# Tail scores moved next to the next pair's first scores, with a new order in the early pairs

## The chip, the cores and the metric

The kernel runs on one core of a Trainium2 chip. The metric is the device time of one execution in microseconds. TensorE (PE), VectorE (DVE), ScalarE (ACT) and GpSimd (POOL) each run their own instruction stream in order; SyncE (SP) issues the DMAs. Streams wait for each other by semaphores alone.

## What is computed

Attention with a memory over 4 x 8 heads of 576 rows and 64 columns, then two expert layers on the 2304 rows of 512, all in float32:

```python
scores = scale * q @ k.T, causal;  a = softmax(scores)
local = a @ v
mem_out = (phi(q) @ M_prev) / (phi(q) @ z_prev + 1e-6)
x = g * mem_out + (1 - g) * local          # rows x 512 over the heads

h = x @ w_in                               # 512 x 1024
solu = h * softmax(h);  ln = (solu - mu) / sqrt(var + 1e-6) * g_ln
x = ln @ w_out                             # 1024 x 512

out = (sigmoid(x @ w_gate) * (x @ w_val)) @ w_out2
```

## The kernel before, in words

Everything is written out by hand: each engine's block holds its operations in the order in which they run, and semaphores with counts tie the blocks together. The work has three stages.

**Early pairs.** Heads are taken two at a time, 16 pairs g. Pairs 0 to 4 run alone (`early_step`, L1455 on PE, L743 on ACT, L1011 on DVE). A pair's 576 query rows are cut in tiles of 128 and a tail of 64; with two heads there are nine score tiles in seven units (`UNITS`), issued in four batches: `scores(g, 0)` to `scores(g, 3)`. Batch 3 is the tail of both heads (`TAIL_TILE`); it also reads `turned`, a copy of q's and k's tail with the heads swapped, loaded by DMA for each pair. Per unit DVE adds the mask, finds the row maximum and copies the tile out (`unit_max`, L905); ACT takes the exponential (`exp_tile`, L588); DVE scales by one over the sum, in three parts (`normalize`, L916). In the step of the next pair PE transposes the probabilities in seven fills (`turn_p`, L1349), each copied from one of two banks by `keep_pt` (L595 on ACT, L949 on DVE); fill n waits for the copy of fill n - 2. `memory` (L1405) makes the memory's part, `scale_memory` (L931) scales it on DVE, `feature` (L913) makes phi(q). One step later again, `weighted` (L1364) sums memory and weighted values, and ACT's `keep_x` (L602) puts them into `xT`.

Between these, ACT and DVE split the weights of the first expert in a high and a low part: `split_w1` for the four quarters of w_in (L606, L953), `split_w2` for the eight blocks of w_out (L611, L958), in places given by tables (`W1_LO_MEM` and so on). The raw weights lie in a part of `xT`. So SP loads w_out (L476, eight DMAs of 256 KB) only when all four low quarters of w_in are done (`sp.wait_ge(w1_lo_ok, DC)` after its step 3), and q, k (L417, L420), `turned` (L433, L435) and v of the next pairs stand behind those loads in the same queue.

**Joint steps.** From pair 5 on, `step(g, t)` puts the attention of pair g beside tile t = g - 5 of the first expert (t = 0 to 11; at t = 11 there is no pair left). `moe_x` (L616, ACT) and `split_x` (L546, POOL) split x of a tile into high and low; `moe_hidden` (L1420) is three products for each of the eight (block, half) pairs into the two banks `m_bk`; DVE's `moe_max`, ACT's `moe_exp` and DVE's `moe_rows` (L971) turn h into rows, after which `m_bk` is free; `moe_var`, `rstd` on POOL (L551) and `moe_norm` (L1001) normalize them. In the next step PE transposes the rows (`moe_transpose`, L1430), ACT and DVE split them (`moe_ln` L633, `moe_ln_low` L1008), and `moe_out` (L1444) multiplies by w_out. `moe_out_t` (L1451) transposes the result, and DVE's `moe_store_x` (L988) stores it. `OWN` holds the tiles (0 and 4) whose x is complete only within their own step.

Units 0 and 1 of the scores lie in `s_bk` banks 0 and 1, as does the tail (L213), except in pair 0. In a joint step the tail scores stand between transposes and the second half of `moe_out` (L1521), and the next step's first batch behind `moe_out`.

**Behind the steps** six tiles of the first expert are left; the second expert (L1552 to L1605, half of the time) starts among the last of them.

## Time and profile before

| | us |
|---|---|
| median of 3 runs | 845.45 (845.44 to 846.02) |
| the profiled execution's own time | 845.53 |
| its span in the trace | 843.5 |
| PE busy | 816.5 (97%) |
| DVE busy | 601.1 (71%) |
| ACT busy | 466.3 (55%) |
| POOL busy | 39.0 (5%) |
| chain that ended last: PE / DVE / ACT / issue | 90% / 5% / 2% / 2% |

Pairs 0 to 4 take the first 64 us, the joint steps go from 64 to 338, the six tiles to about 425, the second expert to the end. Times in a timeline are from the span's start. A row gives start, length, engine, line, operation, what is written from what, how many were merged, and in brackets the idle time just before with the engine or DMA that ended it. A row's length reaches to the last result; the distance between two starts is what an instruction costs its engine. "PEclk" is the granted clock of TensorE, 1.00 for 2.4 GHz and 0.50 for 1.2 GHz.

### The profile page before, as it was taken

How to read it: one execution, taken by the hardware profiler on the slowest of the kernel's cores; microseconds unless marked ns; L12 is line 12 of the kernel's file. 1: busy time of each engine (PE TensorE's matmuls, PEld its weight loads, DVE VectorE, ACT ScalarE, POOL GpSimd, SP SyncE). 2: the span in 40 equal slices, each digit the busy share in tenths (PEclk: the TensorE clock that was granted, in tenths of full speed). 3: DMA queues.
4: the chain of work that ended last, by engine and by line, in shares of the span. 5: the costliest groups of instructions: out<-in, count | busy, mean ns of one | idle time of the engine just before them, and what ended most of it. 6: DMA issues, size and time to landing. Idle time of an engine off the chain costs nothing.

```text
span 843.5 us, 15401 instructions
## 1 busy us (share of the span) xinstructions
PE 816.5 (97%) x5704; PEld 686.0 (81%) x5704; DVE 601.1 (71%) x1447; ACT 466.3 (55%) x965; POOL 39.0 (5%) x47
## 2 busy tenths in 40 slices
PE   5888999999999999999999999999999999999997
PEld 3555777777777777878889999999999999999996
DVE  6988877777777775588565777687676678666653
ACT  6987666666566663364444444574444465444442
POOL 1000000000000001111000000000000000000000
PEclk8999999999999999999999999999999999999999
DMA  7353011111111000100224111103111113111002
GB/s 219 91 171 88 18 53 54 53 54 54 47 44 54 26 18 15 51 1 1 75 54 148 51 51 51 51 26 125 50 51 51 51 27 125 51 51 50 26 1 76
DMA packets 67034, 49.51 MB, mean 59 GB/s; under 512 B 9360, under 2 KB 57488, under 8 KB 66960
## 3 DMA queue, kind: packets, MB, share of 16 engines
q1 hardware_dynamic: 66960, 48.53, 19.3%
q8 instruction: 46, 0.75, 0.4%
q14 instruction: 28, 0.23, 0.1%
HBM read 43.79 MB, written 4.72 MB: 58 GB/s over the span
## 4 chain that ended last, share of the span: by engine, by line
PE 90%; DVE 5%; issue 2%; ACT 2%; SPq 1%; DMA 1%; POOL 0%; DVEq 0%; ACTq 0%
PE tt_bk L1554 10%; PE tt_bk L1552 10%; PE tt_bk L1553 10%; PE m_bk L1420 10%; PE s_bk L1444 7%; PE tt_bk L1349 5%; PE s_bk L1290 4%; PE o_bk L1357 4%; PE o_bk L1444 4%; PE s_bk L1604 3%; PE s_bk L1605 3%; PE s_bk L1603 3%; PE m_bk L1604 2%; PE m_bk L1605 2%; PE m_bk L1603 2%
## 5 line engine op out<-in xcount | busy, mean ns | idle before, releaser
L1554 PE MATMUL tt_bk<-xc_hi,wc_lo 128*128 128x384 f32 x476 | 160.0, 336 | 0.0
L1552 PE MATMUL tt_bk<-xc_hi,wc_hi 128*128 128x384 f32 x476 | 159.9, 336 | 0.0
L1553 PE MATMUL tt_bk<-xc_lo,wc_hi 128*128 128x384 f32 x476 | 159.8, 336 | 0.0
L588 ACT ACTIVATE p_nat<-p_nat,negmax 128x512 f32<-128x512 f32 (+2 forms) x144 | 83.0, 579 | 53.3 <-DVE negmax L905 53.3
L1133 DVE TENSOR_TENSOR wc_lo<-wc_raw,wc_hi 128x768 fp32r<-128x768 f32 x72 | 78.3, 1088 | 32.0 <-ACT wc_hi L653 32.0
L1552 PEld LDWEIGHTS tt_bk<-xc_hi,wc_hi 128*128 128x128 f32 x476 | 89.4, 188 | 6.1
L1553 PEld LDWEIGHTS tt_bk<-xc_lo,wc_hi 128*128 128x128 f32 x476 | 89.4, 188 | 6.1
L1554 PEld LDWEIGHTS tt_bk<-xc_hi,wc_lo 128*128 128x128 f32 x476 | 89.4, 188 | 0.0
L905 DVE CUSTOM_DVE_ANT_0 p_nat<-s_bk,mask 128x384 f32<-128x384 f32 (+2 forms) x124 | 54.9, 489 | 19.4 <-PE s_bk L1290 18.9
L653 ACT CAST wc_hi<-wc_raw 128x768 fp32r<-128x768 f32 x72 | 64.5, 946 | 3.1 <-DVE wc_raw L1127 3.1
L1349 PE MATMUL tt_bk<-ident,p_nat 128*128 128x128 f32 x400 | 56.6, 277 | 7.6 <-ACT pT L595 7.4
L595 ACT COPY pT<-tt_bk 128x512 f32<-128x512 f32 (+1 forms) x87 | 45.7, 552 | 31.9 <-PE tt_bk L1349 30.3
L1349 PEld LDWEIGHTS tt_bk<-ident,p_nat 128*128 128x128 f32 x400 | 46.7, 142 | 20.2 <-issue 13.4
L1290 PE MATMUL s_bk<-qkT 64*64 64x512 f32 (+3 forms) x496 | 47.7, 473 | 9.4 <-DMA qkT<-in_k 4.9
L1420 PE MATMUL m_bk<-w_hi,x_hi 128*128 128x512 f32 x120 | 50.5, 421 | 1.2 <-issue 1.2
L929 DVE TENSOR_SCALAR p_nat<-p_nat,c_loc 128x512 f32<-128x512 f32 (+2 forms) x144 | 50.1, 405 | 1.7
L690 ACT ACTIVATE gv_b<-tt_bk 128x384 f32<-128x384 f32 x34 | 16.7, 492 | 55.3 <-PE tt_bk L1554 55.3
L1420 PE MATMUL m_bk<-w_hi,x_lo 128*128 128x512 f32 x120 | 47.1, 392 | 0.0
L1420 PE MATMUL m_bk<-w_lo,x_hi 128*128 128x512 f32 x120 | 46.8, 390 | 0.0
L1149 DVE TENSOR_TENSOR c_u<-c_u,tt_bk 128x384 f32<-128x384 f32 x34 | 18.8, 553 | 37.4 <-ACT c_u L685 37.3
L700 ACT CAST gv_hia<-gv_a 128x384 fp32r<-128x384 f32 x36 | 18.5, 513 | 39.4 <-DVE gv_a L1164 39.4
L675 ACT ACTIVATE gv_a<-c_p 128x384 f32<-128x384 f32 x36 | 18.9, 526 | 36.3 <-DVE c_p L1144 36.3
(215 smaller groups left out, 1781.1 us busy)
## 6 DMA issues: line engine op xcount, KB each, us to landing
wc_raw<-in_moe_w_val SPq DMA_DIRECT2D x36, 256.0 KB, 3.0
wc_raw<-in_moe_w_gate SPq DMA_DIRECT2D x36, 256.0 KB, 3.4
qkT<-in_q SPq DMA_DIRECT2D x16, 288.0 KB, 2.8
qkT<-in_k SPq DMA_DIRECT2D x16, 288.0 KB, 3.2
v_raw<-in_v SPq DMA_DIRECT2D x16, 256.0 KB, 2.7
out<-o_sb SPq DMA_DIRECT2D x15, 256.0 KB, 2.5
w_raw<-in_moe_w_out SPq DMA_DIRECT2D x12, 256.0 KB, 4.5
turned<-in_k SPq DMA_DIRECT2D x32, 72.0 KB, 2.5
```

Source lines behind the costliest of these rows:

```text
L588: nc.scalar.activation(p_tile(g, tile), p_tile(g, tile), ACT.Exp, bias=negmax[:, n:n + 1], scale=-1.0, accum_out=den[:, n:n + 1]).then_inc ...
L653: nc.scalar.copy(wc_hi[n % 2][:, k, :, :], wc_raw[n % NR][:, r, :, :]).then_inc(wc_hi_ok, 1)
L905: last = nc.vector.tensor_tensor_reduce(out=to, in0=s_tile(g, tile), in1=m, scale=-SCALE, scalar=3.0e38, op0=ALU.add, op1=ALU.min, accum_o ...
L929: nc.vector.tensor_scalar(p, p, c_loc[:, t:t + 1], None, ALU.mult).then_inc(p_ok, 1)
L1133: nc.vector.tensor_tensor(wc_lo[n % 2][:, k, :, :], wc_raw[n % NR][:, r, :, :], wc_hi[n % 2][:, k, :, :].bitcast(F32), ALU.subtract).then_ ...
L1290: last = mm(s_tile(g, tile)[c * D:c * D + D, :], qkT[r, g % 2, 0, a:a + D], qkT[r, g % 2, 1, 0:keys(tile)], start=True, stop=True, skip_gr ...
L1349: last = nc.tensor.transpose(bank[:, c * P:(c + 1) * P], p_nat[g % 2][:, p_at[tile] + j * P:p_at[tile] + (j + 1) * P], ident[:, :])
L1420: last = mm(h_banks(even)[:, n, :], x[:, b, :], w[:, b, c], start=m % (3 * DC) == 0, stop=m % (3 * DC) == 3 * DC - 1)
L1444: last = mm(y_bank(tail), ln[:, f * P:(f + 1) * P], w[:, f, :], start=m == 0, stop=m == 3 * FB - 1)
L1552: mm(o, hi[:, k, c, :], xc_hi[:, j, c, :], start=start and c == 0, stop=False, skip_group_check=True)
L1553: mm(o, hi[:, k, c, :], xc_lo[:, j, c, :], start=False, stop=False, skip_group_check=True)
L1554: last = mm(o, lo[:, k, c, :], xc_hi[:, j, c, :], start=False, stop=c == 1, skip_group_check=True)
```

## The change

- **Joint steps (t from 1, pair from 6).** The tail scores go to `m_bk` and are issued after the whole of `moe_out`, right in front of the next pair's first batch. They wait for the rows of tile t (`u_ok`); the next first batch waits for six maxima of the pair, no longer seven; `weighted` waits for the seventh. On ACT the tail's exponential moves behind `moe_y`, on DVE its maximum behind `moe_norm`.
- **split_x** of the tiles up to 12 goes from POOL to DVE, except tile 4.
- **Early pairs.** PE issues scores 1 between the main part and the tail of `weighted`, and fills 2, the memory, 3 and 4 after scores 2. ACT copies fills 0 to 2 before exponentials 2 and 3, and fills 3 to 6 before exponentials 4 and 5 and the weights. DVE's first normalization, the maxima 4 to 6 and the two memory scalings are in a new order; `split_w1` of `W1_LO_MEM` stands behind the second scaling, which is now behind the tail's maximum, and `feature` comes last but for the weights of `W1_LO_PHI`.
- **t = 11:** the transposes of tile 10 come first, then `weighted`, then `moe_out_t`; ACT and DVE split the turned rows before they keep or normalize on.
- **Behind the steps:** for tile 12 `moe_ln` and `moe_ln_low` stand one place earlier, before the square and the variance of tile 13.

```diff
@@ -209,8 +209,9 @@
...

+
             if tile == TAIL_TILE:
-                return (s_bk if g else m_bk)[:, 0:2, 0:HALF]
+                return (m_bk if g == 0 or g > M0 else s_bk)[:, 0:2, 0:HALF]
             u = [tile in unit for unit in UNITS].index(True)
...
@@ -550,14 +551,13 @@
...

-            def step(g):
-                if g >= M0:
-                    rstd(g - M0)
-                if g >= M0 - 1:
-                    split_x(g - M0 + 1)
-
-            for g in range(PAIRS + 1):
-                step(g)
+            def step(g, t):
+                if t and t in OWN:
+                    split_x(t)
+                rstd(t)
+
+            for g in range(M0, PAIRS + 1):
+                step(g, g - M0)

...
@@ -744,25 +744,27 @@
...
                 if g > 1:
-                    keep_both(g - 2)
+                    keep_x(g - 2, 0)
                 if g:
                     keep_pt(g - 1, 0)
+                if g > 1:
+                    keep_x(g - 2, 1)
+                if g:
                     keep_pt(g - 1, 1)
-                for n in range(2, 6):
+                    keep_pt(g - 1, 2)
+                exp_tile(g, 2)
+                exp_tile(g, 3)
+                if g:
+                    for n in range(3, NF):
+                        keep_pt(g - 1, n)
+                for n in range(4, 6):
                     exp_tile(g, n)
-                if g:
-                    keep_pt(g - 1, 2)
-                    keep_pt(g - 1, 3)
                 for c in W1_HI_MID.get(g, ()):
...
                 exp_tile(g, 7)
-                if g:
-                    keep_pt(g - 1, 4)
-                    keep_pt(g - 1, 5)
-                    keep_pt(g - 1, 6)
                 feature_relu(g + 1)
...
@@ -775,10 +777,10 @@
...
                     exp_tile(g, 1)
-                if t > 1 and g < PAIRS:
+                if t > 1:
                     moe_ln(t - 1)
                 keep_both(g - 2)
-                if t == 1 or g == PAIRS:
+                if t == 1:
                     moe_ln(t - 1)
...
@@ -805,8 +807,6 @@
...
                     keep_pt(g - 1, 6)
-                if t and g < PAIRS:
-                    exp_tile(g, 8)
                 for f in W2_HI_END.get(g, ()):
...
@@ -815,6 +815,8 @@
...
                     moe_y(t - 1)
+                if t and g < PAIRS:
+                    exp_tile(g, 8)

...
@@ -837,10 +839,12 @@
...
             moe_y(t, True)
+            moe_ln(t + 1)
             moe_square(t + 2)
...
                 even = (i - t) % 2 == 1
-                moe_ln(i)
+                if i > t + 1:
+                    moe_ln(i)
                 if i == t + 1:
...
@@ -959,6 +963,11 @@
...

+            def split_x(t):
+                dve.wait_ge(x_hi_ok, t + 1)
+                nc.vector.tensor_tensor(x_lo[:, :, :], xT[:, :, bass.ds(t * P, P)],
+                                        x_hi[:, :, :].bitcast(F32), ALU.subtract).then_inc(x_lo_ok, 1)
+
             def moe_max(t, even=False):
...
@@ -1016,20 +1025,21 @@
...
                 unit_max(g, 3)
+                normalize(g, 0)
+                unit_max(g, 4)
+                unit_max(g, 5)
                 if g:
                     scale_memory(g - 1, 0)
+                unit_max(g, 6)
+                if g:
                     scale_memory(g - 1, 1)
...
                         split_w1(c)
-                unit_max(g, 4)
-                unit_max(g, 5)
                 feature(g)
...
                     split_w2(f)
-                unit_max(g, 6)
-                normalize(g, 0)

...
@@ -1038,17 +1048,17 @@
...
                 normalize(g - 1, 1)
-                if t > 1 and g < PAIRS:
+                if t:
                     moe_ln_low(t - 1)
...
                     moe_store_x(t - 2)
-                if t == 1 or g == PAIRS:
-                    moe_ln_low(t - 1)
                 if g < PAIRS:
...
                     unit_max(g, 3)
+                if t == 0:
+                    split_x(t)
                 if t == 1:
...
@@ -1078,10 +1088,12 @@
...
                     split_w2(W2_LO_TILE[g][2])
+                moe_var(t)
+                moe_norm(t)
+                if t + 1 not in OWN:
+                    split_x(t + 1)
                 if t and g < PAIRS:
                     unit_max(g, 6)
-                moe_var(t)
-                moe_norm(t)

...
@@ -1236,12 +1248,14 @@
...
             moe_stats(t + 2)
-            low_xc(0, B21)
+            moe_ln_low(t + 1)
             moe_var(t + 2)
             moe_norm(t + 2, False)
+            low_xc(0, B21)
             for i in range(t + 1, TILES):
                 even = (i - t) % 2 == 1
-                moe_ln_low(i)
+                if i > t + 1:
+                    moe_ln_low(i)
                 if i + 2 >= TILES:
...
@@ -1296,13 +1310,15 @@
...
                     pe.wait_ge(k_in, 16 * g + 16)
-                    wait(pe, max_ok, NU * g if g > 1 else 2 * g)
+                    wait(pe, max_ok, NU * g - 1 if g > M0 + 1 else NU * g if g > 1 else 2 * g)
                 elif g == 0:
...
                     pe.wait_ge(max_ok, NU * g + 3)
+                elif g > M0:
+                    pe.wait_ge(u_ok, g - M0 + 1)
                 else:
...
@@ -1361,7 +1377,7 @@
...

-            def weighted(h):
+            def weighted_main(h):
                 wait(pe, x_ok, 2 * h)
...
@@ -1379,10 +1395,16 @@
...
                 last.then_inc(o_ready, 1)
+
+            def weighted_tail(h):
                 for j in range(ST):
...
                 last.then_inc(o_ready, 1)
+
+            def weighted(h):
+                weighted_main(h)
+                weighted_tail(h)

...
@@ -1455,16 +1477,19 @@
...
                 if g > 1:
-                    weighted(g - 2)
+                    weighted_main(g - 2)
                 scores(g, 1)
+                if g > 1:
+                    weighted_tail(g - 2)
                 if g:
...
                     turn_p(g - 1, 1)
-                    memory(g - 1, None)
                 scores(g, 2)
                 if g:
-                    for n in range(2, 5):
-                        turn_p(g - 1, n)
+                    turn_p(g - 1, 2)
+                    memory(g - 1, None)
+                    turn_p(g - 1, 3)
+                    turn_p(g - 1, 4)
                 scores(g, 3)
...
@@ -1473,10 +1498,7 @@
...
                     scores(g, 0)
-                if g == PAIRS:
-                    pe.wait_ge(u_ok, t)
-                    weighted(g - 2)
-                if t > 1:
+                if 1 < t and g < PAIRS:
                     moe_out_t(t - 2)
...
@@ -1485,8 +1507,10 @@
...
                     pe.wait_ge(u_ok, t)
-                if g < PAIRS:
-                    weighted(g - 2)
+                pe.wait_ge(max_ok, NU * g)
+                weighted(g - 2)
+                if g == PAIRS:
+                    moe_out_t(t - 2)
                 if t == 1:
...
@@ -1517,10 +1541,10 @@
...
                 turn_p(g - 1, 6)
+                if t:
+                    moe_out(t - 1, 12, 24)
                 if t and g < PAIRS:
                     scores(g, 3)
-                if t:
-                    moe_out(t - 1, 12, 24)

...
```

## Rows read from the trace of the kernel before

**Rows 1.** Stretches, length, busy us (instructions) by engine, granted clock, DMA share, GB/s.
```profile
9.60:11.70 2.10, 0.00 (x0) 0.00 (x1) 2.10 (x10) 2.10 (x9) 0.00 (x0) 1.00 1.00 379
11.70:13.50 1.80, 1.72 (x8) 0.23 (x8) 1.62 (x6) 1.80 (x6) 0.00 (x0) 0.60 1.04 421
...
50.80:64.20 13.40, 11.10 (x159) 7.19 (x158) 11.69 (x43) 11.54 (x31) 0.00 (x0) 1.00 0.77 231
107.90:131.10 23.20, 23.20 (x219) 17.38 (x219) 17.19 (x55) 14.63 (x36) 2.14 (x3) 1.00 0.17 49
```

**Rows 2.** Timelines of PE and DVE in joint steps: scores, memory, transposes, products, maxima.
```profile
136.97 1.09 PE L1290 MATMUL s_bk<-qkT 64*64 64x384 f32 x16
137.88 0.76 PE L1405 MATMUL tt_bk<-mz,phi 64*64 64x66 f32 x40
...
150.17 0.49 PE L1349 MATMUL tt_bk<-ident,p_nat 128*128 128x128 f32 x3
150.59 0.46 PE L1322 MATMUL s_bk<-qkT 64*64 64x288 f32 x2
...
154.21 1.09 PE L1290 MATMUL s_bk<-qkT 64*64 64x512 f32 x8
155.23 0.66 PE L1451 MATMUL s_bk<-ident,y_nat 128*128 128x128 f32 x4
...
334.84 0.49 PE L1349 MATMUL tt_bk<-ident,p_nat 128*128 128x128 f32 x3
335.08 0.48 PE L1444 MATMUL s_bk<-w_hi,ln_hi 128*128 128x512 f32 x1
...
151.49 0.76 DVE L905 CUSTOM_DVE_ANT_0 p_nat<-s_bk,mask_tail 128x576 f32<-128x576 f32 x1 [1.29 <-PE s_bk L1326]
...
155.47 0.69 DVE L905 CUSTOM_DVE_ANT_0 p_nat<-s_bk,mask 128x512 f32<-128x512 f32 x1 [1.31 <-PE s_bk L1290]
```

**Rows 3.** Timelines of DVE and POOL: normalizations in steps t = 1, 3.
```profile
88.06 2.16 DVE L929 TENSOR_SCALAR p_nat<-p_nat,c_loc 128x384 f32<-128x384 f32 x4
...
134.54 1.14 DVE L929 TENSOR_SCALAR p_nat<-p_nat,c_loc 128x384 f32<-128x384 f32 x4
...
88.31 1.30 POOL L546 TENSOR_TENSOR x_lo<-xT,x_hi 128x512 fp32r<-128x512 f32 x1 [1.79 <-ACT x_hi L616]
```

**Rows 4.** Timelines of DVE and PE in t = 11 and at tile 12.
```profile
320.83 0.69 DVE L988 TENSOR_SCALAR xT<-s_bk 128x512 f32<-128x512 f32 x1 [0.29 <-PE s_bk L1451]
...
323.27 0.81 PE L1405 MATMUL tt_bk<-mz,phi 64*64 64x66 f32 x40 [1.61 <-issue]
...
367.05 0.50 PE L1444 MATMUL o_bk<-w_hi,ln_hi 128*128 128x512 f32 x1 [0.70 <-DVE ln_lo L1008]
```

**Rows 5.** Timeline of DVE in pair 3.
```profile
47.04 1.21 DVE L953 TENSOR_TENSOR w_lo<-xT,w_hi 128x1024 fp32r<-128x1024 f32 x1
...
48.86 0.75 DVE L913 SCALAR_TENSOR_TENSOR phi<-qexp,qrelu 128x576 f32<-128x576 f32 x1
...
50.62 0.88 DVE L929 TENSOR_SCALAR p_nat<-p_nat,c_loc 128x512 f32<-128x512 f32 x2
```

**Rows 6.** DMA issues, landing of the one at 55.17, PE, ACT in pair 4.
```profile
48.28 3.66 SPq L476 DMA_DIRECT2D xT<-in_moe_w_out  x8
...
55.17 1.30 SPq L435 DMA_DIRECT2D turned<-in_k  x1
...
DMA to landing us min/median/max: 6.0/6.0/6.0
...
61.29 0.46 PE L1322 MATMUL s_bk<-qkT 64*64 64x288 f32 x2
...
59.95 0.95 ACT L595 COPY pT<-tt_bk 128x512 f32<-128x512 f32 x2
```

**Rows 7.** Timelines of ACT and PE at x of tile 0.
```profile
70.53 0.62 ACT L616 CAST x_hi<-xT 128x512 fp32r<-128x512 f32 x1
...
72.69 0.47 PE L1420 MATMUL m_bk<-w_hi,x_hi 128*128 128x512 f32 x1 [1.17 <-issue]
```

## The prediction, as put down before the changed kernel was run

> **What bounds the kernel now.** I read the table of stretches first, then the timelines of TensorE, VectorE, ScalarE and the DMA queue, stretch by stretch. In a joint step (a pair's attention beside a tile's first expert, some 23.2 us each) TensorE is busy for 23.20 of 23.20 us, while VectorE and ScalarE have 6 and 8.6 us to spare [rows 1]. No wait is left there to remove: only TensorE's own instruction stream can get shorter. In the early pairs it is otherwise: in pair 4 (50.8 to 64.2) TensorE is busy for 11.1 of 13.4 us, and VectorE and ScalarE for 11.7 and 11.5 [rows 1]. Three engines and the DMA queue hand on to each other there, and a reordering moves waits.
>
> **Joint steps: scores beside scores.** Before, the tail scores (64x64 blocks) stand between transposes and 128x128 products, and the next pair's first scores again behind products. After, they are neighbours. Three transposes take 0.42 us up to the start of tail scores (150.17 to 150.59) but 0.24 us up to a product (334.84 to 335.08): the edge costs 0.18. The first batch takes 1.02 us (154.21 to 155.23) where a 128x128 transpose follows, and the second batch, with as many columns, 0.91 (136.97 to 137.88) where the memory's 64x64 blocks follow: 0.11 for the edge out [rows 2]. One such pair of edges goes away: 0.29 us a step. Bounds: 0.15 (one edge alone) and 0.4. It holds for 9 steps (t = 1 to 9; pair 15 has no successor): 9 x 0.29 = **2.6 us off** (1.3 to 3.6), and 0.1 in t = 10.
>
> What could eat it: the tail's maximum now comes right in front of the next pair's first maxima. VectorE starts that maximum 0.9 us after the tail scores (150.59 and 151.49) and needs 0.7; a first batch's maximum starts 1.26 us after the batch (154.21 and 155.47) [rows 2]. Tail scores start some 0.55 before the batch, so VectorE is through at 1.05, about 0.2 early. The new wait in front of the weighted products comes 2.4 us after the first batch's start, over 1 us after that maximum. The tail scores wait for the rows of the same tile, done over 4 us earlier. Each costs nothing while those margins hold. The exponential of the tail on ScalarE ends within 0.1 us of where the next pair's first one could begin. The low half of x, 0.6 us on VectorE, lies in its spare 6 us.
>
> **Step t = 1.** VectorE now makes the low half of tile 1's x, and first waits for ScalarE's high half (about 0.65 us), then works 0.6. Against it: the four normalizations of this step took 2.16 us beside GpSimd's own low half, 1.14 in t = 3 [rows 3], so 1.0 comes back. Net **0.3 us later** on the way to the low half of the turned rows, for which the memory batch already waits; 1.3 if the 2.16 has another cause. The Trainium skill (SBUF: State Buffer, Who interferes with whom) says that VectorE and GpSimd share one port pair, that copies and tensor_scalar in VectorE's two-port modes take it, and that the later one blocks fully. By that rule the price is 0.3 and not 1.3, and the rows, with GpSimd at work from 88.31 to 89.61, agree with it.
>
> **t = 11 and behind.** The memory batch stood still for 1.61 us, the low half of the turned rows being late [rows 4]. After, transposes lead, and that half comes early. What is late next: x's store of tile 9, which waits for the transpose behind the weighted products and stands behind both normalizations; it takes 0.7 us (320.83) and the handing over another 0.2. So **0.8 us off**, not 1.6. One tile on, TensorE waited 0.70 us for the same kind of half [rows 4]; with the move it is there 2.5 us earlier: **0.75 us off**; VectorE's chain behind it also moves by 0.8, so the gain survives.
>
> **Early pairs: what the reordering moves.** Locally it helps. Tail scores no longer wait for five maxima that sit behind memory scaling, and by hand TensorE reaches the starts of pairs 2, 3 and 4 some 1.4 us earlier. But one more step is moved: VectorE's low quarter of w_in in pair 3 (L953) stood right behind the memory scaling and ended at 48.25. After, it follows the first normalization, two maxima and the tail's maximum too. From 48.25 to 51.50 VectorE does just these, with the feature step (0.7) between: 3.25 - 0.7 = 2.6 us (rounded up) more in front of it [rows 5]. Besides, in pair 1 a low quarter then waits for its high quarter, which ScalarE now does behind four copies and two exponentials: about 1.2 us of idle VectorE, of which 0.6 is left by pair 3. So that quarter ends at 48.2 + 2.6 + 0.6 = 51.4.
>
> On the DMA queue the eight loads of w_out wait for exactly this quarter (48.28), and behind them in the same queue stand q, k and the turned tail of pair 4. The last turned load is issued at 55.17, lands 6.0 us later, at 61.2, and the tail scores start at 61.29: there is no slack already [rows 6]. All of it shifts by 3.2: the turned tail lands at **64.4**. TensorE, early, has nothing but those scores to do from about 59.7 on, and idles for 4.7 us. ScalarE idles too: its copies 5 and 6 wait for transposes behind those scores, and behind the copies now stand exponentials and five blocks of w_out. From its copy 2 at 59.95 to the end of x's high half at 71.15 it took 11.2 us with 0.2 idle; without copies 2, 3 and 4 (1.3) and with exponentials 4 and 5 (1.0) about 10.6 us lie between copy 5 and x [rows 6, 7].
>
> The clock: TensorE idled 2.1 us (9.6 to 11.7), and in the stretch from there the granted clock is 0.60, falling to the lower level of 1.2 GHz; eight score records took 1.72 us instead of 1.09 [rows 1, 2]. A hole of 4.7 us will do the same, I take it: tail scores 1.2 and four transposes 1.0. Copy 5 starts at 64.4 + 2.2 + 0.2 = 66.8, x's high half ends at 77.4, VectorE's low half (0.6; it must wait) is there at 78.1, and the first hidden product, at 72.69 before [rows 7], starts at 78.1: 5.4 later. With 0.2 of VectorE's backlog by the end of the step: **5.6 us later**. Bounds: 4.4 (clock stays up, loads shift by 3.2) and 7.5 (the low clock reaches into the products of t = 0); if nothing is late, 2 us below nothing.
>
> **Sum.** 845.53 (the profiled execution's own time) + 5.6 + 0.3 - 2.6 - 0.1 - 0.8 - 0.75 = 847.2. That execution lies 0.1 above the median of 845.45, so 847.1 as a median.
>
> **Rivals.**
> *Early gain.* The loads are not late, or not missed. Decides: whether the w_in quarter ends before about 49 us, so that the turned tail is there at 62. Then the early pairs give what the reordering is for: 1.4 us at the start of pair 4, up to 2 at t = 0. Against it: the quarter is behind 2.6 us more work on an engine busy for 11.7 of 13.4 us. Time: 845.45 - 2 + 0.3 - 4.25 = 839.5; with a half effect 842. This one ends faster.
> *Clock stays up.* The hole is shorter or ends in time; copy 5 starts 1.2 earlier: 845.9.
> *No edge saved.* Neighbouring scores still cost the same (the quadrants of the tail differ in kind), or the tail's maximum makes each next pair late by as much: all else as forecast, 847.1 + 2.6 = 849.7. For it: margins of 0.1 to 0.2 us on VectorE. Against: memory behind scores shows the edge gone.
> *Long slow clock.* Products of t = 0 at half speed for 2 us more: 849.1.
> The Trainium skill (TensorEngine Tiling, Key Properties) states that a change of tiling mode drains TensorE; by it each change of block size left out saves time. The 0.18 and the 0.11 agree with it [rows 2], so "no edge saved" has the smaller chance.
>
> **Chances.** Forecast 0.42; early gain 0.23; clock stays up 0.13; no edge saved 0.12; long slow clock 0.10. Of these, faster by over 0.2% (1.7 us, about what a measurement of this kernel tells from no change) holds the early gain and a little of the second: 0.26. Slower by over 0.2% holds half of the forecast and the last two: 0.43. The forecast lies just at that border, so within 0.2% keeps 0.31. The likeliest case's own range is 845.0 to 848.8; the range that holds 8 in 10 reaches down to the half early gain and up to the last two: 841.5 to 849.8.
>
> **What the next profile would show.** The w_in quarter of pair 3 ending near 51.4, w_out loads issued from there, tail scores of pair 4 at 64.4 behind a hole of some 4 us on TensorE with a drop in the granted clock behind it, and the first hidden product near 78. If these scores start before 62, the early part is wrong. Joint steps of 22.9 instead of 23.17 us show the edges; 23.17 or more refutes them. In t = 1 the four normalizations should take 1.14. In t = 11 the memory batch should follow the store of x with no other wait.

## The result and the profile after

Over 11 runs each, the changed kernel takes **847.95 us** (846.60 to 850.01) and the kernel before 845.45 us (845.05 to 846.06): a ratio of 1.0031, 95% interval 1.0022 to 1.0040. The change makes the kernel 0.3% slower. The changed kernel is also less steady: 3.4 us lie between its fastest and its slowest run, against 1.0 before.

The page of the changed kernel (profiled execution 848.55 us, its span 846.8; before 845.53 and 843.5):

```profile
span 846.8 us, 15410 instructions
PE 816.9 (96%) x5704; PEld 687.9 (81%) x5704; DVE 606.7 (72%) x1459; ACT 465.6 (55%) x965; POOL 20.7 (2%) x35
...
PE   5877899999999999999999999999999999999998
PEclk8998999999999999999999999999999999999999
...
PE 88%; DVE 5%; ACT 3%; issue 2%; DMA 1%; SPq 1%; POOL 0%; DVEq 0%; ACTq 0%
```

TensorE is 0.96 busy; the first slices, up to some 85 us, are the ones that aren't full. Its waits, longest sum first (line, waited for, sum, times, longest):

```profile
PE s_bk L1304 <- DVE negmax L909: 7.5, 12, 1.4
PE s_bk L1338 <- DMA turned<-in_k: 4.4, 1, 4.4
...
PE o_bk L1466 <- DVE ln_lo L1017: 0.9, 1, 0.9
PE tt_bk L1427 <- DVE xT L997: 0.8, 1, 0.8
```

The 4.4 us for the turned rows are a new wait. The 0.9 us for `ln_lo` stand at tile 13, where 0.70 us stood at tile 12 before [rows 4]. The memory batch of t = 11 stands still for 0.8 instead of 1.6 us [rows 4]. The early part, now as a timeline (start, length, engine, line, out<-in, idle before it):

```profile
50.93 1.22 DVE L957 TENSOR_TENSOR w_lo<-xT,w_hi 128x1024 fp32r<-128x1024 f32 x1
52.17 4.77 SPq L477 DMA_DIRECT2D xT<-in_moe_w_out  x8
59.90 0.60 SPq L436 DMA_DIRECT2D turned<-in_k  x1
DMA to landing us min/median/max: 4.4/4.7/4.9
64.96 0.46 PE L1338 MATMUL s_bk<-qkT 64*64 64x288 f32 x2 [4.44 <-DMA turned<-in_k]
66.76 1.12 ACT L595 COPY pT<-tt_bk 128x512 f32<-128x512 f32 x2 [5.43 <-PE tt_bk L1365]
76.84 0.62 ACT L616 CAST x_hi<-xT 128x512 fp32r<-128x512 f32 x1
78.28 0.47 PE L1442 MATMUL m_bk<-w_hi,x_hi 128*128 128x512 f32 x1 [1.90 <-issue]
...
80.56 0.63 PE L1442 MATMUL m_bk<-w_lo,x_hi 128*128 128x512 f32 x1
```

The quarter of w_in starts at 50.93 instead of 47.04 [rows 5], the w_out loads wait for it, the last turned load lands at 64.8 instead of 61.2 [rows 6], and the first hidden product starts at 78.28 instead of 72.69 [rows 7]. The last row is a hidden product at half speed: from start to start these take 0.43 instead of 0.23 us. The granted clock by stretch (length, busy us of TensorE, weight loads, VectorE, ScalarE and GpSimd, granted clock, DMA share, GB/s):

```profile
60.50:65.00 4.50, 0.06 (x5) 0.07 (x5) 0.45 (x1) 0.83 (x2) 0.00 (x0) 1.00 0.85 259
65.00:69.50 4.50, 4.50 (x26) 2.17 (x27) 2.19 (x6) 2.69 (x8) 0.00 (x0) 0.62 0.48 130
75.00:78.30 3.30, 0.68 (x9) 0.26 (x9) 2.13 (x11) 3.27 (x11) 0.00 (x0) 1.00 0.18 41
79.20:83.20 4.00, 4.00 (x18) 2.55 (x16) 3.72 (x12) 2.57 (x9) 0.00 (x0) 0.57 0.00 0
```

Twice TensorE idles (4.44 of 4.5 us, then 2.6 of 3.3) and twice the clock falls to 1.2 GHz behind it; 0.62 and 0.57 are means over stretches that hold some time at 2.4 GHz too. Later parts, against [rows 2], [rows 3] and [rows 4]:

```profile
96.49 1.14 DVE L933 TENSOR_SCALAR p_nat<-p_nat,c_loc 128x384 f32<-128x384 f32 x4
...
115.49 1.04 PE L1304 MATMUL s_bk<-qkT 64*64 64x512 f32 x8
138.33 1.04 PE L1304 MATMUL s_bk<-qkT 64*64 64x512 f32 x8
...
111.96 0.50 PE L1466 MATMUL s_bk<-w_hi,ln_hi 128*128 128x512 f32 x1 [0.24 <-DVE w_lo L962]
...
327.47 0.75 PE L1427 MATMUL tt_bk<-mz,phi 64*64 64x66 f32 x35 [0.78 <-DVE xT L997]
370.32 0.48 PE L1466 MATMUL o_bk<-w_hi,ln_hi 128*128 128x512 f32 x1
383.88 0.50 PE L1466 MATMUL o_bk<-w_hi,ln_hi 128*128 128x512 f32 x1 [0.94 <-DVE ln_lo L1017]
```

Two neighbouring first batches are 22.84 us apart; before they were 23.16 (131.05 and 154.21). The row at 111.96 is the second half of the output products in t = 1, which waits for a low block of w_out from VectorE.

**Where it went.** How far the changed kernel is behind, in the two profiled executions:

| point on TensorE | before | after | behind |
|---|---|---|---|
| first batch of pair 2 | 24.38 | 23.54 | -0.84 |
| first batch of pair 5 (t = 0) | 64.17 | 67.29 | +3.12 |
| first hidden product | 72.69 | 78.28 | +5.59 |
| first batch of pair 6 (t = 1) | 83.21 | 90.42 | +7.21 |
| memory of t = 1 | 91.47 | 98.89 | +7.42 |
| first batch of pair 7 | 107.88 | 115.49 | +7.61 |
| first batch of pair 15 | 293.51 | 298.43 | +4.92 |
| memory of t = 11 | 323.27 | 327.47 | +4.20 |
| output products of tile 12 | 367.05 | 370.32 | +3.27 |
| output products of tile 13 | 379.65 | 383.88 | +4.23 |
| last evacuation on VectorE | 837.92 | 842.17 | +4.25 |
| end of the span | 843.5 | 846.8 | +3.3 |

### The profile page after: what moved, and what is told of

Its sections match the earlier page's. It is cut to its first block, busy times and chain, and to the rows that moved or that the text cites. A ratio compares the mean times of both kernels' runs of the same rounds, so it can differ in the third digit from the quotient of the medians.

```text
span 846.8 us, 15410 instructions
## 1 busy us (share of the span) xinstructions
PE 816.9 (96%) x5704; PEld 687.9 (81%) x5704; DVE 606.7 (72%) x1459; ACT 465.6 (55%) x965; POOL 20.7 (2%) x35
## 4 chain that ended last, share of the span: by engine, by line
PE 88%; DVE 5%; ACT 3%; issue 2%; DMA 1%; SPq 1%; POOL 0%; DVEq 0%; ACTq 0%
PE m_bk L1442 10%; PE tt_bk L1578 10%; PE tt_bk L1576 10%; PE tt_bk L1577 10%; PE s_bk L1466 7%; PE tt_bk L1365 4%; PE o_bk L1466 4%; PE s_bk L1304 3%; PE s_bk L1628 3%; PE s_bk L1629 3%; PE s_bk L1627 3%; PE o_bk L1373 3%; PE m_bk L1628 2%; PE m_bk L1629 2%; PE s_bk L1442 2%
## 5 line engine op out<-in xcount | busy, mean ns | idle before, releaser
L1304 PEld LDWEIGHTS s_bk<-qkT 64*64 64x64 f32 x496 | 16.7, 139 | 33.2 <-issue 17.1
```

The costliest lines, as they stand in the source:

```text
L1304: last = mm(s_tile(g, tile)[c * D:c * D + D, :], qkT[r, g % 2, 0, a:a + D], qkT[r, g % 2, 1, 0:keys(tile)], start=True, stop=True, skip_gr ...
```

## The experiments

Two theories stood against each other for the early part. *Queue:* w_in's quarter is late, the DMA queue with it. *Order:* the new order of the handings-over is slower by itself. A third, the *clock*, says how much of the loss is TensorE at half speed. For the rest the question was whether the saved edges are real and why the gain at tile 12 didn't last. The kernel before was timed again beside each of the three groups of kernels (medians 845.48, 845.74 and 845.24 us), and each ratio is against its own; so medians of two groups can be compared to some 0.5 us.

**1. Early part and the rest, taken apart.** `old_early` is the changed kernel with `early_step` of ScalarE, VectorE and TensorE as before; `new_early_only` is the kernel before with only these functions new.

```diff
 old_early:       after.py,  early_step (ACT, DVE, PE) <- before.py
 new_early_only:  before.py, early_step (ACT, DVE, PE) <- after.py
                  (weighted cut in two, as early_step needs it)
```

> The changed kernel with the early pairs' order of the kernel before on TensorE, VectorE and ScalarE; joint steps, t = 11 and tile 12 as changed. It gives what the other parts are worth: by the steps of the prediction 845.45 + 0.3 - 2.6 - 0.1 - 0.8 - 0.75 = 841.5; with the gain at tile 12 given back at tile 13, as the trace of the changed kernel shows, 842.2. If the joint steps give nothing, 844.5 or more.

> The kernel before with the early pairs' order of the change alone. Theory: the whole loss is here, 845.45 + 5.6 (as predicted) to + 7.2 (as the changed kernel's trace has it): 851 to 853, with runs several microseconds apart. If early and other parts interact, it is under 850.

Measured: `old_early` **840.37 us** (839.90 to 841.25), ratio 0.9941 (0.9929 to 0.9954); `new_early_only` **854.26** (852.95 to 854.55), ratio 1.0101 (1.0085 to 1.0116). The early part alone costs 7.6 us (847.95 - 840.37) to 8.8 (854.26 - 845.48), and all the rest saves 5.1 (845.48 - 840.37) to 6.3. Both halves are larger than I had expected (840.37 against 841.5 or 842.2, 854.26 against 851 to 853). That the two ways of taking apart differ by 1.2 us lies in the start-up, as far as the four traces tell: counted from the first batch of pair 2 on, the early part costs 8.5 or 8.7 us and the rest saves 4.3 or 4.5. Some 0.9 us of what the rest saves is the landing of the last stores (see the end).

**2. The queue.** Two repairs of the changed kernel, and the one late quarter in the kernel before:

```diff
 low_first:    early_step, DVE
                 unit_max(g, 3)
+                for c in W1_LO_MEM.get(g, ()): split_w1(c)
                 normalize(g, 0)
...
                 scale_memory(g - 1, 1)
-                for c in W1_LO_MEM.get(g, ()): split_w1(c)
 turned_first: SP issues q, k and the turned rows of the pair whose
               loads queued behind w_out ahead of the w_out loads
 quarter_late: before.py, DVE, pair 3 only
                 scale_memory(g - 1, 1)
-                split_w1(3)
...
                 normalize(g, 0)
+                split_w1(3)
```

> The changed kernel, with VectorE's low quarter of w_in in pairs 2 and 3 in front of the first normalization, two places earlier than in the change. Theory (queue): the late quarter holds back the w_out loads, and these the turned tail of pair 4. The quarter of pair 3 should end near 47.5 us (52.1 in the changed kernel), the w_out loads start there, the hole in front of the tail scores of pair 4 shrink from 4.4 us to under 1, the granted clock stay at its upper level, the first hidden product start near 73.5 instead of 78.3, and the time be 841 to 842. Rival (order): the new early order itself costs the time, whatever the loads do: 847 to 848, first hidden product later than 76.

> The changed kernel, with only the DMA queue reordered: q, k and the turned tail for pairs 5 and 4 are issued ahead of the eight w_out loads, which still wait for the late quarter of w_in. Theory (queue): the tail scores of pair 4 no longer wait for a DMA although the quarter is as late as before; hole under 1 us, time 841 to 842.5. If the w_out blocks themselves are what comes late, ScalarE waits for them behind and the time lies at 843 to 845. Rival (order): 847 to 848.

> The kernel before (845.45 us), with one edit of the change alone: in pair 3 the third quarter of w_in (1.21 us on VectorE) stands behind the unit maxima and the first normalization instead of in front of them. Theory of the queue: the w_out loads start when it ends, about 3.5 us later, q, k and the turned rows of the fourth pair queue behind them and land at about 64.5 instead of 61.2, the tail scores of the fourth pair wait for them, and the pair behind starts 2 to 3.5 us later: 847.5 to 849. Rival, that the wait falls on time that VectorE and ScalarE need anyway (they are over 0.9 busy there): 845.5 to 846.2.

Measured: `low_first` **842.81 us** (841.70 to 845.06), ratio 0.9973 (0.9963 to 0.9984); `turned_first` **844.12** (842.31 to 845.74), 0.9985 (0.9976 to 0.9993); `quarter_late` **848.30** (847.38 to 849.61), 1.0034 (1.0022 to 1.0047), 3.06 us over its kernel before. The late quarter in the kernel before:

```profile
50.36 1.22 DVE L953 TENSOR_TENSOR w_lo<-xT,w_hi 128x1024 fp32r<-128x1024 f32 x1
51.60 3.67 SPq L476 DMA_DIRECT2D xT<-in_moe_w_out  x8
63.89 0.75 PE L1326 MATMUL s_bk<-qkT 64*64 64x288 f32 x2 [3.99 <-DMA turned<-in_k]
66.75 1.98 PE L1294 MATMUL s_bk<-qkT 64*64 64x512 f32 x8
```

The same tail scores in `low_first` and in `turned_first`, without a wait:

```profile
58.66 0.46 PE L1338 MATMUL s_bk<-qkT 64*64 64x288 f32 x2
```
```profile
59.85 0.46 PE L1343 MATMUL s_bk<-qkT 64*64 64x288 f32 x2
```

One VectorE instruction of 1.22 us, moved, makes the tail scores of pair 4 wait 3.99 us for the DMA. So the queue costs 3.1 us in the old order and 5.1 in the new one (847.95 - 842.81), where the same quarter is late. The order-only theory (847 to 848 for `low_first`) is refuted. But `low_first`, at 842.81, misses the 841 to 842 that I had expected, and is still 2.4 us behind `old_early`, which the queue doesn't explain. (Its quarter doesn't only go back: it ends at 45.36, earlier than the 48.25 of the kernel before.) `turned_first` lies in the 843 to 845 that I had given to the case that ScalarE waits for late w_out blocks; its trace shows no such wait, so that reason is not confirmed. It reaches pair 5 0.8 us later than `low_first` (table below), and why wasn't followed.

**3. What is left without the queue.** Times on TensorE of each kernel's profiled execution, from the first batch of pair 2 on, since the start-up before it varies:

| kernel | pair 2 at | to pair 5 | pair 5 to first hidden product | pair 5 to pair 6 |
|---|---|---|---|---|
| before | 24.38 | 39.79 | 8.52 | 19.04 |
| quarter_late | 23.57 | 43.18 | 8.53 | 19.08 |
| old_early | 24.71 | 39.81 | 8.02 | 18.56 |
| after | 23.54 | 43.75 | 10.99 | 23.13 |
| low_first | 22.55 | 37.92 | 10.91 | 23.04 |
| lead | 24.39 | 38.47 | 8.32 | 19.98 |
| lead_old_clear | 23.47 | 39.78 | 8.02 | 19.67 |
| hole_filled | 22.59 | 43.01 | 10.89 | 23.83 |
| low_first_wide | 24.75 | 37.90 | 10.91 | 21.45 |
| low_first_filled | 23.36 | 37.98 | 10.91 | 23.02 |
| turned_first | 22.93 | 38.73 | 10.92 | 23.04 |
| new_early_only | 24.30 | 43.52 | 11.70 | 23.83 |

Without the queue's hole the new order is 1.9 us faster to pair 5 (37.92 against 39.81). All of that comes in pair 4, which takes 11.34 instead of 13.40 us; by the start of pair 4 nothing is gained (26.58 against 26.41 from pair 2 on). Step t = 0 then takes 4.5 us more (23.04 against 18.56): 2.9 ahead of the first hidden product and 1.6 behind it, where the clock is low (experiment 4). Together 2.6 us are lost, which fits the 2.4. The 2.9 are ScalarE's: from the copies at 66.76 to x's high half at 76.84 (rows of after, above) it works 10.1 us without a pause, through seven exponentials, two feature activations and five w_out blocks. `lead` is `low_first` with that order changed in t = 0, `lead_old_clear` the same on `old_early` (with the wait of `tail_clear`, below):

```diff
 lead: step(g, 0), ACT
+                keep_both(3); moe_x(0)
                 exp_tile(5, 0); exp_tile(5, 1)
+                w_out splits of W2_HI_END[4]   (from the end of early_step(4))
-                keep_both(3); moe_x(0)
       step(g, 0), DVE
                 normalize(4, 1)
-                normalize(4, 2)
                 unit_max(5, 2); unit_max(5, 3); split_x(0)
+                normalize(4, 2)
```

> The changed kernel with the w_in quarters ahead of the first normalization (842.81 us), and in the first joint step ScalarE copies the weighted rows and x_hi before the w_out splits and the first two exponentials (3.3 us of work ahead of it moved behind), and VectorE does the second normalization behind x_lo. Theory that the queue of ScalarE ahead of x_hi is what is left of the early loss: x_hi ends at about 67.3 instead of 70.5, the first hidden product starts at 68.9 to 69.5 instead of 71.4, the clock stays up: 838.5 to 840. Rival, that the moved work (w_out splits, exponentials) is needed as early by the next step's turns and outputs: the hidden products start early but the step ends where it did, 842 to 843.

> The candidate for the fastest version: the changed kernel with the early pairs in their old order, the first joint step with x_hi ahead of the w_out splits and exponentials on ScalarE, and the wait of tail_clear on GpSimd. If the three savings add up: x_hi some 1.5 us earlier, of which 1.0 is left at the next step, and 0.8 at tile 13: 838.5. If the first joint step ends where it did since its later copies come later, 839.6; if neither edit brings anything beside the old early order, 840.4.

Measured: `lead` **841.00 us** (839.73 to 841.32), ratio 0.9944 (0.9931 to 0.9956), 1.8 us under `low_first` and between the two theories: 838.5 to 840 if ScalarE's queue is all, 842 to 843 if the moved work is needed as early. The trace shows both. The hidden products start 2.6 us earlier behind pair 5 (8.32 against 10.91), and the clock stays up, which is worth 1.6; but the time from there to pair 6 is only 0.5 us shorter (11.66 against 12.13), so 1.1 us are lost again to late maxima and copies. `lead_old_clear` **840.66** (840.24 to 841.54), ratio 0.9946 (0.9933 to 0.9958): no gain, and 0.9 us over `tail_clear`, which is the same without it; the intervals overlap, but t = 0 is longer by 1.1 us in the trace (19.67 against the 18.56 of `old_early`). The hidden products start no earlier there (8.02 both): x's high half is done at 68.84, but VectorE makes the low half only behind its four maxima, from 70.48. And the normalization that was moved behind the low half makes other maxima late:

```profile
75.24 0.46 PE L1345 MATMUL s_bk<-qkT 64*64 64x288 f32 x2 [0.97 <-DVE negmax L917]
```

**4. The clock.** Three ways to keep TensorE from idling, with products that are done again or whose result nobody reads:

```diff
 hole_filled:      after, in front of the tail scores of pair 4
+   7 x the tail's two QK products (64x288), before the turned_in wait
 low_first_filled: low_first, memory part of t = 0
+   its 40 products of 66 columns three times more
 low_first_wide:   low_first, memory part of t = 0
+   10 products of 128x512 into the free turning bank
```

> The changed kernel (847.95 us), with seven more copies of the tail's two QK products (64x288) put in front of the wait for the turned rows in the fourth head pair, so that TensorE isn't idle in the 4.4 us before its tail scores. Nothing else moves. If the granted clock falls because of that idle stretch, it now stays at 1.00 from 65 to 70 us, and the slow stretch (65 to 69.5 us, 4 us at about half) gives back about 1.8 us: 846.1. The second idle stretch (75.7 to 78.3) and the fall behind it are left. If the clock falls whatever TensorE does there, the time is 848.0 or, if a product still runs when the rows land, 848.3. If the clock of the first stretch hid nothing because VectorE and ScalarE set the end there, the clock is 1.00 and the time is still 848.

> The changed kernel with the w_in quarters ahead of the first normalization (842.81 us), and here the products of the memory part of the first joint step are done four times instead of once (3 x 0.76 us more, where TensorE otherwise waits for maxima and for x_lo, 66.8 to 71.4 us). Nobody waits for their result before 71.2. If idle time is what makes the clock fall at 71.9, it stays at 1.00 and the twelve products behind it take 2.9 us instead of 4.5: 841.2 (at most 0.2 of it lost to a later third batch of scores). If the fall comes from something else, 842.8 to 843.0.

> The changed kernel with the w_in quarters ahead of the first normalization (842.81 us), and ten dummy products of 128x512 into the free turning bank in front of the memory part of the first joint step (10 x 0.23 us, 65.9 to 68.3, where TensorE otherwise waits for maxima). Few long products instead of 120 short ones, so that the stretch is filled to about 69.5. If the clock's fall behind 71.4 comes from that idle stretch, the granted clock stays at 1.00 and the twelve hidden products take 2.9 instead of 4.5 us: 841.2. If the 1.9 us of idle time right ahead of the hidden products are enough to bring the fall, 842.8.

Measured: `hole_filled` **849.17 us** (847.28 to 849.43), ratio 1.0035 (1.0023 to 1.0048): nothing gained on the 847.95 of the changed kernel, and none of my three cases (846.1, or 848.0 to 848.3) met. `low_first_filled` **842.89** (841.56 to 843.70), 0.9966 (0.9954 to 0.9979). `low_first_wide` **842.76** (841.04 to 842.87), 0.9964 (0.9950 to 0.9978). The stretches, first of `hole_filled`, then of `low_first`, then of `low_first_wide` (columns as above):

```profile
66.00:69.00 3.00, 3.00 (x31) 1.78 (x25) 2.22 (x4) 3.00 (x10) 0.00 (x0) 1.00 0.67 222
...
75.00:78.00 3.00, 1.51 (x4) 1.26 (x5) 2.16 (x8) 2.61 (x10) 0.00 (x0) 0.50 0.00 0
78.00:81.00 3.00, 3.00 (x9) 2.35 (x8) 2.93 (x11) 1.92 (x6) 0.00 (x0) 0.50 0.00 0
```
```profile
66.00:69.00 3.00, 0.95 (x52) 0.81 (x48) 2.93 (x13) 3.00 (x7) 0.00 (x0) 1.00 0.43 115
69.00:72.00 3.00, 1.09 (x10) 0.54 (x5) 1.78 (x8) 2.97 (x11) 0.00 (x0) 0.97 0.00 0
72.00:75.00 3.00, 3.00 (x8) 2.34 (x7) 2.86 (x13) 1.57 (x9) 0.00 (x0) 0.50 0.00 0
```
```profile
69.00:72.00 3.00, 3.00 (x57) 1.97 (x55) 2.58 (x12) 3.00 (x8) 0.00 (x0) 1.00 0.25 74
72.00:75.00 3.00, 1.51 (x10) 1.24 (x7) 2.10 (x7) 2.67 (x10) 0.00 (x0) 1.00 0.06 11
75.00:78.00 3.00, 3.00 (x19) 1.88 (x18) 2.93 (x11) 1.86 (x6) 0.00 (x0) 1.00 0.00 0
```

In `hole_filled` the clock did stay at 1.00 behind the first hole, and pair 5 came 0.74 us earlier (43.01 against 43.75), but behind the second hole the clock was low for longer (0.50 in both stretches) and t = 0 took 0.7 more. In this pair of traces the fall removed in one place was paid in the next. In `low_first_wide` the clock stays up and t = 0 is 1.6 us shorter (21.45 against 23.04), just the price of about eight of the twelve hidden products running at 0.43 instead of 0.23 us from start to start. Its median (842.76, the same as that of `low_first`) shows nothing of this, though. The profiled execution had lost as much at start-up: pair 2 starts 2.2 us later than in `low_first` (clock 0.61 from 12 to 25 us, 0.87 in that of `low_first`). What the second fall costs a median stays open, between nothing and 1.6 us. `low_first_filled` missed its aim: with 157 of its 160 short products done, TensorE stood still by itself,

```profile
70.91 0.27 PE L1436 MATMUL tt_bk<-mz,phi 64*64 64x66 f32 x2 [1.55 <-issue]
```

so that it made the hole it should have filled, and the clock fell as before (t = 0 takes 23.02 us).

**5. The edges.** `tail_apart` is `old_early` with the tail scores back in the middle of the output products, in the score banks, and their maximum and exponential where they were.

```diff
 tail_apart: step(g, t), PE
+                scores(g, 3)
                 moe_out(t - 1, 12, 24)
-                scores(g, 3)
```

> The kernel with the early pairs in their old order (840.37 us), and the tail scores of the steps with tiles put back where they stood, in the score banks in the middle of the output products. If the saving of a joint step (23.17 to 22.84 us in the traces) is that merged edge, nine steps lose 0.33 each: 843.3. If a part of it comes from the other edits of a step (the order of the copies and of x_lo), less: 841 to 842.5.

Measured: **843.17 us** (842.87 to 843.57), ratio 0.9970 (0.9960 to 0.9981), 2.8 over `old_early`. First batches of pairs 7 and 8 in `tail_apart`, then in `old_early`:

```profile
107.40 1.09 PE L1301 MATMUL s_bk<-qkT 64*64 64x512 f32 x8
130.57 1.09 PE L1301 MATMUL s_bk<-qkT 64*64 64x512 f32 x8
```
```profile
108.15 1.04 PE L1301 MATMUL s_bk<-qkT 64*64 64x512 f32 x8
130.98 1.04 PE L1301 MATMUL s_bk<-qkT 64*64 64x512 f32 x8
```

23.17 against 22.83 us: the whole saving of a step hangs on the place of the tail scores. The edit moves their bank, their maximum and their exponential along with them, but between these two batches TensorE waits for nothing in either kernel, so it is the order on TensorE that counts. Nine times 0.34 is 3.1; 2.8 is found in the medians, and the move also has its price in t = 1 (below), which `tail_apart` doesn't pay.

**6. Tile 12 to tile 13.** In the changed kernel GpSimd's low half of x for tile 15 and VectorE's low half of a closing operand run side by side:

```profile
372.26 1.28 POOL L547 TENSOR_TENSOR x_lo<-xT,x_hi 128x512 fp32r<-128x512 f32 x1 [3.43 <-ACT x_hi L616]
372.56 1.80 DVE L1126 TENSOR_TENSOR xc_lo<-xc_raw,xc_hi 128x768 fp32r<-128x768 f32 x1
```

`tail_clear` is `old_early` in which GpSimd waits for that operand:

```diff
 tail_clear: POOL, behind the steps
+                pool.wait_ge(xc_lo_ok, 3)
                 split_x(tile 15)
```

> The kernel with the early pairs in their old order (840.37 us), with one wait more: GpSimd starts the x_lo of tile 15 only when VectorE's third split of the closing part's operands has ended. In the traces the two ran side by side (x_lo 364.93 to 366.23, the split 365.22 with 1.81 us instead of 0.95), the rows of VectorE behind it came late, and the output products of tile 13 waited 0.95 us for ln_lo. Theory that this collision took back what the earlier ln_lo of tile 12 had gained: the split takes 0.95, the wait at tile 13 falls to about 0.1, and the time is 839.5 to 839.7. Rival, that VectorE's whole chain from tile 12 to 13 is too long for it anyway: 840.2 to 840.5, with the wait at tile 13 still 0.5 or more.

Measured: **839.76 us** (839.44 to 841.39), ratio 0.9936 (0.9924 to 0.9949). That is 0.6 us under `old_early`, which is within the noise: the two intervals overlap. What shows the collision is the trace:

```profile
364.33 0.95 DVE L1125 TENSOR_TENSOR xc_lo<-xc_raw,xc_hi 128x768 fp32r<-128x768 f32 x1
365.36 1.29 POOL L547 TENSOR_TENSOR x_lo<-xT,x_hi 128x512 fp32r<-128x512 f32 x1 [4.76 <-DVE xc_lo L1125]
...
PE tt_bk L1426 <- DVE xT L997: 0.8, 1, 0.8
PE s_bk L1472 <- ACT y_nat L640: 0.3, 1, 0.3
```

The operand takes 0.95 again, and of TensorE's waits behind 310 us only these two are left; the 0.95 us at tile 13 is gone. `tail_clear` has the lowest median of this study, 0.64% under the kernel before.

## Why the prediction was right

The time came out at 847.95 where 847.1 was forecast, slower by 0.3%. The cause was right: one late quarter, the DMA queue behind it, a hole on TensorE, a low clock, a late x. The chain in the early part held link by link. That the number came out so near is in part luck. In the profiled executions the change costs 3.3 us where 1.65 were added up, and the terms were further off than their sum: the early part cost 1.6 more, tile 12 saved 0.75 less, t = 1 cost 0.4 more and t = 10 and 11 saved 0.2 less; against these stand 0.9 at the last stores and 0.4 at the edges. The profiled execution also lies 0.6 us above the median of its kernel, and had reached pair 2 0.84 us earlier than that of the kernel before.

- **The moved quarter and the DMA queue: right.** Forecast: quarter done at 51.4, turned rows landed at 64.4, a hole of 4.7 us, x's high half done at 77.4, first hidden product at 78.1. Found: 52.1, 64.8, 4.4, 77.5, 78.28. `quarter_late` shows that this one move is the cause, `low_first` and `turned_first` that undoing it by either end of the queue brings 5.1 and 3.8 us back.
- **"5.6 later": too small.** 5.4 by the first hidden product was right (5.59), but "with 0.2 of VectorE's backlog" was wrong: 7.21 us by pair 6. I had let the clock fall once, behind the hole, and given its second fall, behind the wait for x, only as a rival ("long slow clock", 2 us). It came as its own fall, behind its own idle time of 2.6 us. That costs 1.6 us: eight of the first twelve hidden products at 0.43 instead of 0.23.
- **"Clock stays up: copy 5 starts 1.2 earlier, 845.9": it didn't come.** The clock was 0.62 behind the hole. Nor would it have paid so much: `hole_filled` kept the clock up there, pair 5 came 0.74 us earlier, and the time was no better.
- **The local gain of the new order: wrong in place and in what becomes of it.** "1.4 us earlier by hand" at the starts of pairs 2, 3 and 4 was 0.84, 0.69 and 0.45 in the changed kernel: a start-up that was quicker by 0.84, half of it lost again by pair 4. With the queue repaired 1.9 us are gained, but within pair 4. The rival that passed it on ("up to 2 at t = 0", 839.5) would have been wrong even so: `low_first` is at 842.81, for ScalarE's work ahead of x is the same and now in the way.
- **Edges: right, a little small.** 0.29 was forecast for a step, 0.33 found (eight steps from pair 7 to 15: 2.69), so 3.0 instead of 2.6. `tail_apart` shows the place of the tail scores to be the cause. The margins on VectorE held. The Trainium skill (TensorEngine Tiling (Array Packing), Key Properties) states that a change of tiling mode drains the engine. The 0.33 agrees with it; no row shows the draining itself.
- **t = 1: 0.3 was forecast.** 0.2 by the memory batch, and the four normalizations take 1.14 us as said; by pair 7 it is 0.7 (7.61 - 7.21, and one edge of 0.33 saved on the way). The other 0.5 is a wait that the move itself makes, and that the prediction lacks. With the tail scores gone from between the transposes and the second half of the output products, these follow sooner, and need VectorE's low block of w_out (done at 111.91) at once: they start at 111.96, 0.73 us behind the start of the three transposes, where 0.24 would do (the prediction's own row for transposes up to a product). In TensorE's waits it is `w_lo`, 0.2; `old_early` has the same one, `tail_apart` hasn't.
- **t = 10 and 11: right.** 0.9 off was forecast, 0.72 found, with the wait named beforehand (the store of x, 327.47).
- **Tile 12: the gain came and went.** 0.93 us by tile 12, and 0.96 given back by tile 13, so the 0.75 of the forecast came to nothing. The sentence that failed is "VectorE's chain behind it also moves by 0.8, so the gain survives": it moved into GpSimd's work. In [rows 3] I had read the same collision in t = 1, and didn't look for it here. The Trainium skill (SBUF — State Buffer, Who interferes with whom) says that a VectorE instruction with two SBUF inputs contends with one of GpSimd that reads SBUF, and that the one issued first keeps the ports. The rows agree: GpSimd started 0.3 us earlier, and VectorE's 0.95 became 1.80.
- **The end: not forecast.** The span is 0.9 us shorter than the last evacuation tells. The last stores land sooner, and nothing in the prediction speaks of it (see below).

Together: 7.2 + 0.7 - 3.0 - 0.7 + 0.0 - 0.9 = 3.3 in the spans of the profiled executions (3.0 in their times), 2.5 in the medians; forecast were 1.65.

## What to carry to other kernels

Before an instruction is moved on one engine, look for the DMAs that wait for it, and for what is queued behind them: the place of 1.2 us of work decided over 3 to 5 us here. A stretch that gets shorter on one engine is worth only what the next engine's queue lets through, so read the queue ahead of the next hand-over (x's high half) before counting the gain. Where blocks of one size can stand side by side on TensorE, that gain is small (0.33 us), but it is the same in every step and survived everything else. And an instruction can hide a wait where it stands: before it is moved away, look at what the work behind it needs.

## What I had not expected of the hardware

- **The granted clock fell again 14 us after its first fall**, behind an idle stretch of only 2.6 of 3.3 us, and when the first fall was prevented the second lasted longer (0.50 from 75 to 81 us instead of 0.57 from 79.2 to 83.2). In the kernel before, TensorE idled 1.6 us between 70 and 73 us, and the clock stayed at 1.00, in the hidden products behind it too.
- **The start-up differs from execution to execution.** The clock granted between 12 and 25 us was between 0.61 and 1.00 in these profiles. In the old order pair 2 started between 23.47 and 24.71 us, in the new one between 22.55 (clock 0.87) and 24.75 (0.61). The new order hangs more on TensorE there, and that fits the wider spread of its runs: the two slowest of the changed kernel (849.68 and 850.01) have the lowest mean clock of the eleven, 0.988. It wasn't tested by itself.
- **Behind 157 products of 66 columns TensorE stood still for 1.55 us** (`low_first_filled`) with nothing that it waited for in the trace. The cause is open.
- **The last stores.** In the three kernels that keep the old order from the joint steps on (before, `new_early_only`, `quarter_late`) the slowest of the last six stores took 3.0 to 3.2 us to land, in the eleven others 2.1 or 2.2. Of before, then of after:

```profile
DMA to landing us min/median/max: 2.0/2.1/3.0
```
```profile
DMA to landing us min/median/max: 2.0/2.1/2.2
```

That is the 0.9 us at the end. Which edit does it is open: `tail_apart` has the shorter landing too, so it isn't the place of the tail scores.
